# A channel network as seven half-sized products in place of eight, in three token groups and two phases

## The reference

```python
scores = scale * (q @ k.T)          # window of 128 keys, a slope for each head
x = softmax(masked scores + bias) @ v            # (4, 576, 512)
h = x.transpose(0, 2, 1) @ U @ V                 # rank 32, over the tokens
u = x + h.transpose(0, 2, 1)
x2 = u + np.maximum(u @ w_ch1, 0.0) @ w_ch2      # 512 -> 2048 -> 512
h = np.maximum(x2 @ w_in, 0.0)                   # 512 -> 1024, halves u, v
v_n = (v - mean) / sqrt(var + 1e-6)
out = (u * (w_spatial @ v_n + b_spatial)) @ w_out
```

## Time and profile before

| | |
|---|---|
| median of 3 runs | 774.51 us (774.31 to 775.64) |
| profiled execution, its own time | 774.84 us |
| its span, first to last instruction | 773.1 us |
| attention, about | 0 to 155 us |
| channel network, about | 155 to 556 us |
| gated stage, about | 556 to 773 us |
| HBM read and written | 27.83 and 4.72 MB |

### The profile page before, as it was taken

One profiled execution on the slowest core, in us unless ns is written; L12 is line 12 of the kernel. 1 busy time (PEld: TensorE's weight loads), 2 busy tenths in 40 slices (PEclk: granted clock), 3 DMA queues, 4 the chain that ended last, 5 costly groups with the idle time before them and its releaser, 6 DMA issues.

```text
span 773.1 us, 12362 instructions
## 1 busy us (share of the span) xinstructions
PE 758.4 (98%) x4584; PEld 647.9 (84%) x4584; DVE 288.1 (37%) x807; ACT 265.2 (34%) x670; POOL 111.3 (14%) x95
## 2 busy tenths in 40 slices
PE   6999999799999999999999999999999999999998
PEld 4777777578888998888888888888899899998998
DVE  6878777531112113111311113111547417435431
ACT  5877777532322112111210102123343243342422
POOL 1212113344451000000000000123410010100100
PEclk9999999999999999999999999999999999999999
DMA  6333331213322000000000000012100010100101
GB/s 170 111 93 122 93 97 60 82 58 106 109 82 69 1 1 1 1 2 0 1 0 0 0 0 0 27 42 74 56 1 1 20 43 0 46 15 0 61 1 62
DMA packets 24692, 33.04 MB, mean 43 GB/s; under 512 B 2768, under 2 KB 11984, under 8 KB 24656
## 3 DMA queue, kind: packets, MB, share of 16 engines
q1 hardware_dynamic: 24656, 32.56, 13.2%
HBM read 27.83 MB, written 4.72 MB: 42 GB/s over the span
## 4 chain that ended last, share of the span: by engine, by line
PE 96%; DVE 1%; issue 1%; DMA 0%; ACT 0%; POOL 0%; SPq 0%; POOLq 0%; DVEq 0%; ACTq 0%
PE bank L1153 9%; PE bank L1154 9%; PE bank L1152 8%; PE bank L1166 6%; PE bank L1167 6%; PE bank L1168 6%; PE bank L1020 4%; PE wide L1035 3%; PE bank L1002 2%; PE bank L1268 2%; PE bank L1270 2%; PE bank L1269 2%; PE bank L1141 2%; PE bank L1139 2%; PE wide L1167 2%; PE wide L1166 2%
## 5 line engine op out<-in xcount | busy, mean ns | idle before, releaser
L834 DVE SCALAR_TENSOR_TENSOR rl<-bank,rh 128x512 fp32r<-128x512 f32 (+1 forms) x80 | 51.0, 638 | 308.3 <-ACT rh L558 308.3
L558 ACT ACTIVATE rh<-bank 128x512 fp32r<-128x512 f32 (+1 forms) x80 | 44.4, 555 | 312.0 <-PE bank L1154 312.0
L1152 PE MATMUL bank<-uh,w1h 128*128 128x512 f32 (+1 forms) x320 | 118.0, 369 | 0.0
L1153 PE MATMUL bank<-uh,w1l 128*128 128x512 f32 (+1 forms) x320 | 117.9, 368 | 0.0
L1154 PE MATMUL bank<-ul,w1h 128*128 128x512 f32 (+1 forms) x320 | 117.9, 368 | 0.0
L1166 PE MATMUL bank<-rh,w2h 128*128 128x512 f32 (+1 forms) x240 | 88.6, 369 | 0.0
L1168 PE MATMUL bank<-rl,w2h 128*128 128x512 f32 (+1 forms) x240 | 88.4, 368 | 0.0
L1167 PE MATMUL bank<-rh,w2l 128*128 128x512 f32 (+1 forms) x240 | 88.4, 368 | 0.0
L467 ACT ACTIVATE sc<-sc,mn 128x256 f32<-128x256 f32 (+1 forms) x144 | 66.9, 468 | 22.0 <-DVE mn L725 22.0
L1152 PEld LDWEIGHTS bank<-uh,w1h 128*128 128x128 f32 x320 | 60.4, 189 | 10.0
L1154 PEld LDWEIGHTS bank<-ul,w1h 128*128 128x128 f32 x320 | 60.4, 189 | 9.9
(11 more groups left out here) (160 smaller groups left out, 1480.4 us busy)
## 6 DMA issues: line engine op xcount, KB each, us to landing
qkraw<-qk SPq DMA_DIRECT2D x32, 288.0 KB, 3.0
out_t<-tok SPq DMA_DIRECT2D x16, 288.0 KB, 2.1
vraw<-v_n SPq DMA_DIRECT2D x16, 256.0 KB, 2.7
w1raw<-w SPq DMA_DIRECT2D x16, 256.0 KB, 2.9
w2raw<-w SPq DMA_DIRECT2D x16, 256.0 KB, 2.6
w1raw<-w_in SPq DMA_DIRECT2D x8, 256.0 KB, 2.8
w1raw<-w_sp SPq DMA_DIRECT2D x4, 288.0 KB, 2.8
...
```

The lines of the kernel that those rows point to most:

```text
L834: dve.scalar_tensor_tensor(out=rl[:, j % 2, 0:width(c)], in0=r_ps[j % 2][:, 0:width(c)], scalar=0.0, in1=rh[:, j % 2, 0:width(c)], op0=ALU ...
L1152: pe.matmul(o, w1h[:, j, k, :], uh[:, k, 0:w], start=(k == 0), stop=False)
L1153: pe.matmul(o, w1l[:, j, k, :], uh[:, k, 0:w], start=False, stop=False)
```

## The change

The channel network becomes two phases over three groups of 768 tokens. Each group's input is seen as a 2 × 2 block matrix (256 × 2 features by 384 × 2 tokens), w1 and w2 too, and each 2 × 2 block product is made with seven half-sized products (numbered 1 to 7) in place of eight. This needs sums of the blocks of x (T1 to T4), of w1 and w2 (S1 to S4) and of the products.

Phase up: 24 units (3 groups × 8). In a unit s, PE makes seven products of 2 × 3 matmuls of 384 columns, in the order 1, 4 and 3 of the unit before, 2, 6, 5, 7. The products 6, 7 and 4 go on in the bank of product 1, from which ACT has copied out the state before (`keep_p` for 1, 6 and 7, `c21` with relu after 4); 3 goes on in the bank of 5. DVE adds three sums (`c11`, `c12`, `c22`), POOL makes three relus, SP stores the 128 × 4 × 384 block to scratch memory (`store_r`, 0.79 MB a unit). w1 is split and summed into `w1s` for the next units; w2 is split, summed and stored to scratch memory in eight parts (`w2_hi_of`, `w2_sum_of`, `w2_shi_of`, `w2_slow_of`, `w2_low_of`, `store_w2`), in the units 9 to 14, 17 and 18. The six stores of a part read one staging area in `tok`. The input u is stored too (`store_u`).

Phase down: 21 products of 8 parts of 2 × 3 matmuls of 384 columns, each part from a ring of five (`rk`): ACT rounds (`hi_r`), DVE subtracts (`lo_r`), both from SBUF. The r blocks (`load_raw`, `next_raw`), w2's seven forms (`load_w2q`, 128 rows of 16 KB each) and u (`load_u`) come back from scratch memory; POOL makes the T sums of r in halves (`r_sum`; T1 by DVE, `r_sum1`) and adds u (`add_res`); x2 is stored (`store_x2`) and loaded again for the gated stage (`load_x2`). The splits of the weights of the gated stage (`lo_wc` on POOL) move to the end of this phase.

At the start, POOL does `first_w1`, seven `lo_xs` and four `x_sum` of group 0, each over 2 × 384 columns, between its attention work. `c11(0)` writes into `tok`, where group 0's input lies, and so waits for all seven splits.

The core of the diff (`...` for what is left out):

```diff
+G = 3
+HT = TOK // (2 * G)
+UNITS = NF // 2
+NU = G * UNITS
+RING = 5
+QP = 2 * P
...
+UP = []
+for _s in range(NU):
+    UP += [(_s, 1)] + ([(_s - 1, 4), (_s - 1, 3)] if _s else []) + [(_s, m) for m in (2, 6, 5, 7)]
+UP += [(NU - 1, 4), (NU - 1, 3)]
+UP_AT = {x: n + 1 for n, x in enumerate(UP)}
+
+DN = []
+for _g in range(G):
+    DN += [(_g, 1)] + ([(_g - 1, 3), (_g - 1, 4)] if _g else []) + [(_g, m) for m in (2, 6, 5, 7)]
+DN += [(G - 1, 4), (G - 1, 3)]
+DN_AT = {x: (n + 1) * UNITS for n, x in enumerate(DN)}
+ENTRY = {x: n * UNITS for n, x in enumerate(DN)}
+ENTRIES = [(g, m, kk) for g, m in DN for kk in range(UNITS)]
+
+
+W2_UNIT = {9: 0, 10: 1, 11: 2, 12: 3, 13: 4, 14: 5, 17: 6, 18: 7}
+W2_AT = {kk: s for s, kk in W2_UNIT.items()}
...
+            def store_r(s):
+                g, u = divmod(s, UNITS)
+                sp.wait_ge(r_relu, 3 * (s + 1))
+                sp.wait_ge(c21_done, s + 1)
+                sp.dma_start(r_scr[g, u], r_stage(s)).then_inc(r_out[s % 2], 16)
...
+            def store_w2(kk):
+                sp.wait_ge(w2_slow, kk + 1)
+                sp.wait_ge(w2_low, 2 * (kk + 1))
+                for h, parts in ((0, w2_top), (1, w2_bot)):
+                    sp.dma_start(w2_scr[A11, :, h, kk, :], parts[0]).then_inc(w2_out, 16)
+                    q = parts[1] if h == 0 else parts[1].rearrange("p (q c) -> p q c", c=QP)
+                    sp.dma_start(w2_scr[A12:A22 + 1, :, h, kk, :].rearrange("q p c -> p q c"),
+                                 q).then_inc(w2_out, 16)
+                    sp.dma_start(w2_scr[S1:S4 + 1, :, h, kk, :].rearrange("q p c -> p q c"),
+                                 parts[2]).then_inc(w2_out, 16)
...
+            for s in range(NU):
...
+                if s in W2_UNIT:
+                    store_w2(W2_UNIT[s])
+                if s + 1 in W2_UNIT:
+                    load_w2(W2_UNIT[s + 1])
+                if s == LATE + 1:
+                    sp.wait_ge(w2_out, 6 * 16 * UNITS)
+                    sp.wait_ge(xs_lo, 7 * G)
+                    for i in range(2):
+                        sp.wait_ge(r_out[i], 16 * len([n for n in range(LATE) if n % 2 == i]))
+                    for n in "abd":
+                        load_raw(0, n, 0)
+                        load_raw(0, n, 1)
+                for m, ago in ((1, 21), (2, 22), (6, 23)):
+                    if s == ago:
+                        sp.wait_ge(up_p, UP_AT[(s - 2, 3)])
+                        load_w2q(m)
...
+            sp.wait_ge(up_p, UP_AT[(NU - 2, 3)])
+            load_w2q(5)
+            sp.wait_ge(up_p, UP_AT[(NU - 1, 3)])
+            load_raw(0, "c", 0)
+            load_raw(0, "c", 1)
+            store_r(NU - 1)
+            load_w2q(7)
+            load_w2q(4)
+            sp.wait_ge(u_out[0], 16 * G)
+            sp.wait_ge(u_out[1], 16 * G)
+            sp.wait_ge(c11_done, NU)
+            sp.wait_ge(c12_done, NU)
+            sp.wait_ge(c22_done, NU)
+            load_u(0, 11)
+            load_u(0, 12)
...
+            def r_sum(g, m, h):
+
+                u = slice(4 * h, 4 * h + 4)
+                a, b, c, d = (raw[n][:, u, :] for n in "abcd")
+                if m == 3:
+                    pool.wait_ge(raw_in["b"][h], 16 * (g + 1))
+                    pool.wait_ge(raw_in["c"][h], 16 * (g + 1))
+                    pool.tensor_tensor(b, c, b, ALU.subtract).then_inc(rt3, 1)
+                elif m == 2:
+                    pool.wait_ge(rt3, 2 * g + h + 1)
+                    pool.wait_ge(rk_lo, ENTRY[(g, 1)] + 4 * h + 4)
+                    pool.tensor_tensor(a, a, b, ALU.add).then_inc(rt2, 1)
+                else:
+                    pool.wait_ge(rt2, 2 * g + h + 1)
+                    pool.wait_ge(rk_lo, ENTRY[(g, 2)] + 4 * h + 4)
+                    pool.tensor_tensor(d, d, a, ALU.subtract).then_inc(rt4, 1)
+
...
+            def add_res(g, n):
+
+                kept, done, i = {11: (dp1_kept, dp1_u, 0), 12: (du2_kept, du2_u, 1), 22: (du3_kept, du3_u, 2)}[n]
+                pool.wait_ge(u_back[0 if n in (11, 22) else 1], 32 * g + (16 if n != 22 else 32))
+                for m in range(2):
+                    pool.wait_ge(kept, 2 * g + m + 1)
+                    o = sums_d[:, i, m]
+                    pool.tensor_tensor(o, o, u_in[:, 0 if n in (11, 22) else 1, m], ALU.add).then_inc(done, 1)
...
+            for g in range(G):
+                add_res(g, 11)
+                for m in (3, 2, 4):
+                    r_sum(g, m, 0)
+                    r_sum(g, m, 1)
+                if g == G - 1:
+                    for m in range(WU):
+                        lo_wc(m)
+                add_res(g, 12)
+                add_res(g, 22)
...
+            def w2_hi_of(kk):
+
+                act.wait_ge(w2_out, 6 * 16 * kk) if kk else act.wait_ge(xs_lo, 14)
+                for i in range(2):
+                    act.wait_ge(w1_in[i], 16 * (UNITS // 2 + kk + 1))
+                act.activation(w2_top[0].bitcast(F32R), w2_ra[:, 0:QP], ACT.Copy).then_inc(w2_hi, 1)
+                act.activation(w2_top[1].bitcast(F32R), w2_rb.rearrange("p (q c) -> p q c", c=QP),
+                               ACT.Copy).then_inc(w2_hi, 1)
...
+            def keep_p(s, m):
+
+                i, kept, freed = {1: (0, p1_kept, c11_done), 6: (1, u2_kept, c12_done),
+                                  7: (2, u3_kept, c22_done)}[m]
+                act.wait_ge(up_p, UP_AT[(s, m)])
+                if s:
+                    act.wait_ge(freed, s)
+                act.activation(sums_u[:, i, :], a_ps[s % 2][:, 0:HT], ACT.Copy).then_inc(kept, 1)
...
+            step(B - 1, 2)
+            hi_xs(0, 2)
+            hi_xs(0, 6)
+            step(B - 1, 3)
...
+            for s in range(1, NU):
+                g, u = divmod(s, UNITS)
+                keep_p(s, 1)
...
+                if s in W2_UNIT:
+                    w2_hi_of(W2_UNIT[s])
+                c21(s - 1)
...
+                keep_p(s, 6)
...
+                if s in W2_UNIT:
+                    w2_shi_of(W2_UNIT[s])
+                keep_p(s, 7)
...
+            def hi_r(n):
+                g, m, kk = ENTRIES[n]
+                if n >= RING:
+                    act.wait_ge(rk_used, n - RING + 1)
...
+            def w2_slow_of(kk):
+                dve.wait_ge(w2_hi, 3 * (kk + 1))
+                dve.tensor_tensor(w2_bot[2].bitcast(F32R), wst[:, :, :], w2_top[2].bitcast(F32R),
+                                  ALU.subtract).then_inc(w2_slow, 1)
...
+            def c11(s):
+                dve.wait_ge(up_p, UP_AT[(s, 2)])
+                dve.wait_ge(p1_kept, s + 1)
+                if s == 0:
+                    dve.wait_ge(xs_lo, 7)
+                    dve.wait_ge(u_out[0], 16)
+                    dve.wait_ge(u_out[1], 16)
+                room(s)
+                dve.tensor_tensor(r_stage(s, 0), e_ps[:, 0:HT], sums_u[:, 0, :], ALU.add).then_inc(c11_done, 1)
+
...
+            def lo_r(n):
+                g, m, kk = ENTRIES[n]
+                dve.wait_ge(rk_hi, n + 1)
+                dve.tensor_tensor(rk[:, n % RING, 1], raw[RAW_OF[m]][:, kk, :], rk[:, n % RING, 0],
+                                  ALU.subtract).then_inc(rk_lo, 1)
...
+            w1_sum_of(1)
+            c11(0)
+            normalise(B - 1, 3)
...
+            def up(s, m):
+
...
+                elif m == 6:
+                    pe.wait_ge(p1_kept, s + 1)
+                elif m == 7:
+                    pe.wait_ge(u2_kept, s + 1)
...
+                for k in range(2):
                     w = slice(k * P, (k + 1) * P)
-                    pe.matmul(o, w2h[:, j, w], rh[:, j % 2, 0:n], start=(j == 0), stop=False)
-                    pe.matmul(o, w2l[:, j, w], rh[:, j % 2, 0:n], start=False, stop=False)
-                    last = pe.matmul(o, w2h[:, j, w], rl[:, j % 2, 0:n], start=False, stop=(j == NF - 1))
-                if j == NF - 1:
-                    last.then_inc(down_done, 1)
+                    wh, wl = w1s[:, u, 0, WEIGHT[m], w], w1s[:, u, 1, WEIGHT[m], w]
+                    ah, al = xs[:, 0, m - 1, k], xs[:, 1, m - 1, k]
+                    pe.matmul(o, wh, ah, start=(k == 0 and m in FRESH), stop=False, skip_group_check=True)
+                    pe.matmul(o, wl, ah, start=False, stop=False, skip_group_check=True)
+                    last = pe.matmul(o, wh, al, start=False, stop=(k == 1), skip_group_check=True)
+                last.then_inc(up_p, 1)
...
+                for kk in kks:
+                    n = ENTRY[(g, m)] + kk
+                    pe.wait_ge(rk_lo, n + 1)
+                    rh, rl = rk[:, n % RING, 0], rk[:, n % RING, 1]
+                    for e in range(2):
+                        o = {5: dd_ps, 3: dd_ps, 2: de_ps}.get(m, da_ps[g % 2])[e][:, 0:HT]
+                        w = slice(e * P, (e + 1) * P)
+                        wh, wl = w2q[m][:, 0, kk, w], w2q[m][:, 1, kk, w]
+                        pe.matmul(o, wh, rh, start=(kk == 0 and m in FRESH), stop=False, skip_group_check=True)
```

(3 more changed lines are left out.)

1029 lines of the change are left out of this document (738 added, 291 removed).

## The result

The changed kernel takes 902.14 us (median of 4 runs, 900.96 to 904.51), the kernel before 774.73 (774.31 to 775.64): 1.1647 times the time, 95% interval 1.1631 to 1.1663, or 127 us more. The forecast was 864, with a range up to 892. The sign was right; the size was 38 us short.

The account below looks back on a forecast made before the run. PE bounds the kernel, busy 758.4 of 773.1 us. From 774.8: −44.9 matmuls, +2 units, +8 start, +48 w2, +50 handover, +22 lock, +4 end gives 864 (840 to 885 by its bounds; range 805 to 892).

Parts of the forecast that it names:

- Matmuls, −44.9: Channel network on PE: 2,016 matmuls of 384 columns at 0.1731 us take 349.0 us in place of 393.8.
- weight loads set the pace: Rival, PE at 384 columns: weight loads of 0.189 us set matmul spacing, 32 us more, 896; chance 0.03.
- w2, +48: Units 9 to 14, 17, 18: preparation turn of 14.3 us against 7.3 idles PE before product 7; six transitions of 8.
- Handover, +50: From up to down: product 6 waits for T2, behind add_res and u's load on SP's queue; bounds 30 and 65.
- the estimate by the skill's page (40 for the term): Handover: at the skill's 425 GB/s the row of transfers takes 54.6 us, making the term 40.
- The lock, 11 for each of groups 1 and 2: Down phase: DVE gets one lo_r per POOL operation, so T steps starve PE; +22 in all, bounds 0 and 15 per group.
- The lock yields inside a long operation: Rival, down phase: DVE keeps pace beside POOL; −22, and −12 at the handover, giving 830; chance 0.15.
- Start and ordinary units, +10: Start +8, product 7 near 168 not 163 (bounds 3 and 14); ordinary up units 0, w1 and x sums +2.
- Last units of up, 0: Units 22 and 23: late r stores delay c11 by some 3 us, hidden under the handover's wait.
- End, +4: Last two products of down: thirteen POOL subtractions beside lo_r, mostly covered by the ring of five parts; bounds 0 and 8.
- Half clock: After each w2 pause before product 7: slow granted clock costs 1 us more, six transitions.
- The cover holds: Rival, SP's DMA queue: w2 parts and u arrive before asked for, only small terms stay, 744; chance 0.08.

Follow-up runs that it names:

- Experiment 2: Changed kernel with w2 loads issued ahead of the stores and four stores earlier: 892.07 us; that without the three low-part stores: 876.30 us.
- Experiment 1: Changed kernel preparing only four of eight w2 pieces: in units 9 to 12, 880.51 us; spread over units 9, 11, 13 and 17, 862.29 us.
- experiment 3: Changed kernel with group 0's add_res behind its T steps on POOL: 889.74 us; changed kernel with all down-phase T sums on VectorE instead: 876.05 us.
- three moves: Changed kernel with last normalise and last token mix earlier on VectorE, and store of u behind unit 5's w1 load: 897.50 us.
- low parts on VectorE: The kernel with three moves, plus group 0's low parts of x for products 7, 5, 4 and 3 on VectorE, not POOL: 895.43 us.
- experiment 4: Changed kernel with three queue-order moves at the start: 897.50 us; the same with four low parts of x on VectorE: 895.43 us.
- experiment 5: Changed kernel with short w2 chain, VectorE T sums, three start moves, earlier relu of v: 847.67 us; low x parts on VectorE: 845.11; half w2, spread: 807.94.

## Why the prediction was right or wrong

**Matmuls, −44.9: right.** At full clock in the down phase (PE timeline):

```profile
652.76 0.33 PE L1838 MATMUL wide<-rk,w2q 128*128 128x384 f32 x1
...
656.06 0.34 PE L1839 MATMUL wide<-rk,w2q 128*128 128x384 f32 x1
```

19 starts in 3.30 us, 0.174 each; over 226 matmuls from 562 to 601 us it is 39/226 = 0.1726. The line between 288 and 512 columns held. The rival "weight loads set the pace" is out. So did the ones for the copies and sums: ScalarE takes 0.49 for 384 columns, VectorE 0.56.

**w2, +48: mechanism and size right, one part of it missing.** Product 7 stood 5.6 to 7.7 us in six transitions, 39 us, and matmuls at half clock (starts 0.32 apart) cost 10 more in that stretch: 49. By units, the six with a transition lost 52.0; the table's 58.8 also has a group change of 2.6 us and 4.1 in other units. I had 6.0 us to the first store and 8.3 for transfer, issue and landing. In the turn shown it took 6.4 (296.55 to 302.92) and 10.1 (to 312.97), because the r store, 0.79 MB, is in the same turn and was not in the sum; that the size came out all the same is partly luck. Experiment 2 shows the queue moving these short pieces at some 350 GB/s. Experiment 1 shows the chain, experiment 2 that what is on the queue is part of it.

**Handover, +50: order right, rate too low; with the last two units it cost 41.** The queue moved more than the 361 GB/s of the best microsecond before:

```profile
420.00:470.00 50.00, 27.19 (x154) 26.26 (x152) 11.96 (x22) 11.23 (x24) 12.91 (x10) 0.84 0.99 409
```

409 GB/s at a share of 0.99. At that rate my row of 23.2 MB takes 56.7 us and not 64. From the start of unit 20 (398.62), u was there after 65.8 us and not 71, and product 6 was done after 97.4 and not 106. Of the 8.6 us between these, 5.2 are the queue's, 1.9 POOL's steps (3.4 us each and not 3.8), and 1.5 the parts behind them. The Trainium skill, "DMA: Bandwidth & Descriptors", section Bandwidth, has 425 GB/s for loads of 16 MB on one core, issued there by GpSimd; the trace of this stretch, with SyncE's issues, comes near to it, and the estimate by the skill's page (40 for the term) was the better one. The order of steps in the term was as told. That add_res on POOL was the thing in the way is shown by experiment 3 (16 us).

**The lock, 11 for each of groups 1 and 2: right.** Group 1 lost 11.4 us, and group 2 lost 11.0 up to the end of its T steps. lo_r averages 914 ns (the group of 144 above), and beside T steps three took 10.59 us in the kernel of experiment 3, 3.5 each, where 0.56 is its time alone. The Trainium skill, "SBUF — State Buffer", section "SBUF: two separate sides", has the port pair as an exclusive lock; this case now shows it for whole instructions of POOL of 3.4 to 3.9 us, beyond the 1.28 of the earlier trace rows. "The lock yields inside a long operation" is out.

**Start and ordinary units, +10: the step that failed; it cost 34.** The chain of the start was followed as far as product 7 of unit 0, and well: it was put near 168 us and came at 170.2. The units behind it, 1 to 5, were given 0.1 us each for their w1 sums. Lost time by unit:

| units | lost, changed kernel | lost, three moves | lost, and low parts on VectorE |
|---|---|---|---|
| 0 | 12.0 | 12.4 | 10.1 |
| 1 | 5.1 | 5.3 | 7.6 |
| 2 and 3 | 15.0 | 6.7 | 6.8 |
| 4 and 5 | 6.1 | 4.7 | 4.7 |
| 6 to 8 | 3.1 | 5.8 | 2.8 |

So units 1 to 5 lost 26 us, which the sum did not have. The 7.6 us of the kernel before, attention's last transposes and mixes, are in these rows too. What is shown of the 26: the queues were not followed past unit 0. The load of w1 for unit 5 stood behind store_u(2, 0) on SyncE, and add_u behind w1_sum_of(4) on VectorE, two pauses of 9 us together, in units 2 and 3, that went with experiment 4. The lock had been applied to lo_r only, and not to VectorE's w1 sums, which also have two SBUF inputs and ran at 2.0 us in place of 0.42 beside POOL's subtractions; but taking that away gained nothing, so it is not shown to cost. For the other 22 us in units 0 to 5 above the kernel before, the trace shows where they stand, and no experiment says why. The ordinary units themselves were right at 0: units 7 and 20 to 22 lost 0.0 and unit 6 0.5. POOL's relu took 1.17 us alone, under the 1.28 allowed, and 1.475 on average. The two group changes lost 2.6 us each, where 1 was allowed.

**Last units of up, 0: cost 4.4,** and it lies under the handover, as the prediction had it. PE's wait there ends when POOL has T2, behind u on the queue, whenever PE arrives: what PE loses before only shortens the wait. In the kernels of experiments 2 (with six stores) and 4, PE lost 0.2 to 0.9 us more between the start of unit 20 and matmul 1,008, and product 6 started 81.6 to 81.9 us after the start of unit 20 all the same (81.8 in the changed kernel). The table shows it in a row of its own because it counts lost time by the matmul.

**End, +4: cost 18 (12.1 behind the T steps of group 2, and 6.0 in the gated stage).** The three main pauses (POOL, ACT and PE):

```profile
625.80 7.48 POOL L746 TENSOR_TENSOR wvl<-w1raw,wvh 128x512 fp32r<-128x512 f32 x4
...
633.75 0.44 PE L1837 MATMUL bank<-rk,w2q 128*128 128x384 f32 x1 [2.99 <-DVE rk L1407]
...
653.74 2.18 ACT L1044 ACTIVATE wuh<-w1raw 128x512 fp32r<-128x512 f32 x4
655.82 1.81 ACT L1054 ACTIVATE x2h<-tok 128x576 fp32r<-128x576 f32 x3
...
659.31 0.66 PE L1837 MATMUL bank<-rk,w2q 128*128 128x384 f32 x1 [2.91 <-issue]
...
689.11 0.68 ACT L1042 ACTIVATE wsh<-w1raw 128x576 fp32r<-128x576 f32 x1 [2.45 <-DMA w1raw<-w_sp]
...
690.33 0.80 PE L1764 MATMUL wide<-wvh,x2h 128*128 128x512 f32 x1 [4.62 <-ACT vr L1144]
```

The first was in the prediction, and the ring was said to cover most of it: POOL's subtractions for w_in come right behind its last T step and hold up VectorE's lo_r and T1 sum. With the slow matmuls behind it this pause cost 4.8 us. The other two were not in the sum. Seven copies in a row on ScalarE (4.0 us) hold up the rk copies, the ring of five parts is empty when PE comes, and 5.4 us go; that it is these copies is read from the rows, no run moved them. I had looked at POOL's and VectorE's added work there and not at ScalarE's. The last is ScalarE's relu of v behind a split that waits for the last w_sp load: 4.6 us of idle time, and the matmuls after it run at half clock. With the relu moved ahead (experiment 5) it was 1.8.

**Half clock.** I had put 1 us to each of six pauses. Counting all starts 0.28 to 0.36 us apart, the channel stage had 27 us of it: there are 29 pauses above 1.3 us, and 19 of them are followed by 4 to 17 matmuls at 0.32. The row that I had for it was one pause of 3 us. Shorter ones bring it too, but not each: behind five lone pauses of 2.0 to 2.6 us (at 257.7, 363.0, 424.7, 432.0 and 534.5) the matmuls went on at 0.17, and where pauses of 1.7 to 2.6 us came within 2 us of another (484 to 488, 538 to 542, 608 to 612) 4 to 13 matmuls at 0.32 followed. That I had not reckoned with.

**The chances.** "The cover holds" (744) needed all stalls under 45 us; they came to 174. The range was too narrow because each term's upper end was taken from the term's own mechanism (3 to 14 for the start, 0 to 8 for the end), and nothing stood in it for pauses that the terms did not name: start and end hold 38 of the 40 us missed (24 and 14; w2 adds 11, and the handover with the units before it gives 9 back).
